# Attention in front of a mixture of experts: the next iteration's first scores and biases move ahead of the scaling and transposes of the second group

## What is computed

```python
# attention: batch 4, 8 heads, 576 tokens, head size 64; a window of 128 keys
scores = scale * np.matmul(q, k.transpose(0, 1, 3, 2))
bias = slopes[:, None, None] * (-np.abs(rel).astype(np.float32))[None, :, :]
mask = (rel >= 0) & (rel < window)
scores = np.where(mask, scores + bias[None], -1000000000.0)
attn = np.exp(scores - np.max(scores, axis=-1, keepdims=True))
attn = attn / (np.sum(attn, axis=-1, keepdims=True) + 1e-09)
x = np.matmul(attn, v)                      # then (2304, 512)
# mixture of experts: 8 experts, 512 -> 1024 -> 512, all of them for every token
P = np.exp(x @ w_gate - max); 8 rounds of row and column normalisation of P
for e in range(E):
    out += P[:, e:e + 1] * (np.maximum(x @ w1[e], 0.0) @ w2[e])
# feed-forward 512 -> 2048 -> 512 with a leaky relu
return np.maximum(0.01 * h, h) @ w_out      # h = out @ w_in
```

## Time and profile before

| | |
|---|---|
| median of 3 runs | 2029.84 us (2029.77 to 2029.85) |
| the profiled execution | 2029.62 us |
| its span, first to last instruction | 2027.8 us |
| mean granted clock of PE | 1.00 of full speed |
| busy: PE, DVE, ACT, POOL | 2013.9, 1196.0, 625.4, 1170.2 us |
| the chain that ended last: PE, DVE, ACT | 92%, 4%, 3% of the span |

### The profile page before, as it was taken

The page is one execution under the profiler, slowest core; times in us unless marked ns, Lnnn a source line. Parts: engine busy times, 40 slices in busy tenths (PEclk is TensorE's granted clock), DMA queues, the critical chain, the costliest instruction groups (busy, mean ns, idle before and its releaser), DMA issues.

```text
span 2027.8 us, 36541 instructions
## 1 busy us (share of the span) xinstructions
PE 2013.9 (99%) x12584; PEld 1791.1 (88%) x12584; DVE 1196.0 (59%) x2764; ACT 625.4 (31%) x1678; POOL 1170.2 (58%) x1453
## 2 busy tenths in 40 slices
PE   8999999999999999999999999999999999999999
PEld 6679889999998999989899999999999989998998
DVE  7877866555555455566555555555555577667666
ACT  7872232222222222232222222222222243334332
POOL 4425555555565665576555566655555576667551
PEclk9999999999999999999999999999999999999999
DMA  5311111111111111114211111111111115111211
GB/s 175 119 64 43 42 46 49 44 50 41 41 42 51 42 49 44 42 41 117 72 42 52 41 42 41 41 52 41 52 42 41 41 46 128 57 52 56 75 42 47
DMA packets 79891, 113.81 MB, mean 56 GB/s; under 512 B 44352, under 2 KB 53056, under 8 KB 79808
## 3 DMA queue, kind: packets, MB, share of 16 engines
q1 hardware_dynamic: 79808, 112.76, 17.7%
HBM read 103.30 MB, written 9.44 MB: 56 GB/s over the span
## 4 chain that ended last, share of the span: by engine, by line
PE 92%; DVE 4%; ACT 3%; issue 1%; POOL 0%; ACTq 0%; POOLq 0%; DVEq 0%
PE bank L1405 16%; PE bank L1406 16%; PE bank L1407 16%; PE bank L1324 14%; PE bank L1321 14%; PE bank L1323 14%; ACT sc L609 3%; DVE sc L847 1%; DVE sc L832 1%; ACT pt_sb L623 1%; DVE acc L931 0%; DVE row_sum L951 0%; DVE einv L843 0%; DVE esum_eps L841 0%; DVE lt_in L865 0%
## 5 line engine op out<-in xcount | busy, mean ns | idle before, releaser
L942 DVE SCALAR_TENSOR_TENSOR acc<-bank,gate,acc 128x512 f32<-128x512 f32 x495 | 371.6, 751 | 569.2 <-PE bank L1407 569.2
L1324 PE MATMUL bank<-x_hi,up_lo 128*128 128x256 f32 (+1 forms) x2240 | 663.0, 296 | 0.0
L1323 PE MATMUL bank<-x_lo,up_hi 128*128 128x256 f32 (+1 forms) x2240 | 662.4, 296 | 0.0
L1321 PE MATMUL bank<-x_hi,up_hi 128*128 128x256 f32 (+1 forms) x2240 | 661.0, 295 | 0.5 <-DVE hs_lo L1071 0.2
L1406 PE MATMUL bank<-down_lo,hs_hi 128*128 128x512 f32 x1440 | 568.0, 394 | 0.0
L1405 PE MATMUL bank<-down_hi,hs_hi 128*128 128x512 f32 x1440 | 567.5, 394 | 0.4 <-DVE hs_lo L1077 0.4
L1407 PE MATMUL bank<-down_hi,hs_lo 128*128 128x512 f32 x1440 | 560.2, 389 | 0.0
L1321 PEld LDWEIGHTS bank<-x_hi,up_hi 128*128 128x128 f32 x2240 | 423.9, 189 | 30.8 <-DVE bank L1055 1.6
L1323 PEld LDWEIGHTS bank<-x_lo,up_hi 128*128 128x128 f32 x2240 | 423.9, 189 | 24.6
L1324 PEld LDWEIGHTS bank<-x_hi,up_lo 128*128 128x128 f32 x2240 | 423.8, 189 | 0.0
L436 POOL TENSOR_TENSOR up_lo<-stage_up,up_hi 128x256 fp32r<-128x256 f32 x546 | 385.6, 743 | 6.3
(11 more groups left out here) (130 smaller groups left out, 1764.2 us busy)
## 6 DMA issues: line engine op xcount, KB each, us to landing
stage_up<-w_up SPq DMA_DIRECT2D x80, 512.0 KB, 3.5
stage_down<-w_down SPq DMA_DIRECT2D x80, 512.0 KB, 3.5
qk<-qk SPq DMA_DIRECT2D x15, 576.0 KB, 3.7
v_nat<-v SPq DMA_DIRECT2D x16, 320.0 KB, 2.9
x_mem<-x_turned SPq DMA_DIRECT2D x72, 64.0 KB, 2.2
xr<-x_mem SPq DMA_DIRECT2D x16, 256.0 KB, 4.7
result<-acc SPq DMA_DIRECT2D x16, 256.0 KB, 2.7
xr<-x_mem SPq DMA_DIRECT2D x4, 128.0 KB, 4.3
```

Of the source, the lines that this page charges most:

```text
L942: last = d.scalar_tensor_tensor(out=to, in0=y[:, :], scalar=share(g, tile, e), in1=to, op0=ALU.mult, op1=ALU.add)
L1321: m.matmul(to[:, 0:n], up_hi[s][:, w], x_hi[u][:, x], start=first and c == 0, stop=False, skip_group_check=True)
L1323: m.matmul(to[:, 0:n], up_hi[s][:, w], x_lo[u][:, x], start=False, stop=False, skip_group_check=True)
L1324: last = m.matmul(to[:, 0:n], up_lo[s][:, w], x_hi[u][:, x], start=False, stop=c == 1, skip_group_check=True)
```

## The change

Three things change, in the attention iterations alone.

- On PE, S0(i+1) moves from behind T0(i) to directly behind S2(i), ahead of V1(i-1) and T0(i). In iteration 0 twelve keep-busy steps become eight.
- On DVE, B0(i+1) moves from behind N1(i) (and behind the copy of the half logits and, in the last iteration, `sums`) to directly behind B2(i), ahead of N1(i).
- On POOL, `at(i, 0)` waits for N0(i-1) where it waited for N1(i-1). The waits of the groups 1 and 2 stay.

No instruction is added or removed apart from the four keep-busy steps, and ACT's and SP's lists stay as they are. Counts on the semaphores stay the same, since the order among the S, among the B and among the N is kept.

```diff
@@ POOL, at(i, group) @@
-                pool.wait_ge(normed, GROUPS * i + group - 1)
+                pool.wait_ge(normed, GROUPS * i + (-2, 0, 1)[group])
@@ DVE, step @@
                 bias_scores(i, 2, s, pair)
+                if not last:
+                    bias_scores(i + 1, 0, 1 - s, after)
                 normalise(i, 1, s)
                 if half is not None:
                     copy_lt_in(s, half)
                 if last:
                     sums(0, 2)
-                if not last:
-                    bias_scores(i + 1, 0, 1 - s, after)
                 normalise(i, 2, s)
                 if not last:
                     bias_scores(i + 1, 1, 1 - s, after)
@@ PE, step @@
                 scores(i, 2, s)
                 if first:
-                    keep_busy(12)
+                    keep_busy(8)
+                if not last:
+                    scores(i + 1, 0, 1 - s)
                 if not first:
                     values(i - 1, 1, 1 - s)
                 pe.wait_ge(normed, GROUPS * i + 1)
                 transpose_p(0, s)
-                if not last:
-                    scores(i + 1, 0, 1 - s)
                 if not first:
                     values(i - 1, 2, 1 - s)
```

## The result

The changed kernel takes 2038.65 us (median of 6 runs, 2036.78 to 2040.93) against 2029.80 us before: 8.85 us or 0.44% slower, ratio 1.0044 with a 95% interval of 1.0032 to 1.0057. The forecast was 2036.9, in a range of 2032.0 to 2041.6. The profiled execution took 2038.64 us with a span of 2036.9, 9.1 more than before.

A forecast was written before the change was run, and what follows sets the result against it. Attention was taken as bound by a ring of waits E0, C1, E1, N1, B0, replaced by one through B0 of 7.70 us. 107.8 + 1.7 logits + 4.1 POOL, with edges, gave +7.1 us: 2036.9, range 2032.0 to 2041.6.

The forecast's parts named there:

- a second ring that B0 joins: Attention: B1, N0, B2, B0, N1, T1, S1 across DVE and PE; 7.70 us a turn, 6.59 without B0.
- fourteen turns of the ring: Attention, S1 of iteration 1 to S1 of iteration 15: 14 x 7.70 = 107.8 us, against 106.6 before.
- logits ahead of S0: PE: logits queued before S0 make it late by some 0.5 us in iterations 6, 10, 14, 0.1 twice after: +1.7 us.
- POOL at N1: DVE: running POOL instructions hold back N1's L841 through the shared port; sum 3.7 to 4.6 us, taken as 4.1.
- the clock: PE idle before T1 might drop the clock to 1.2 GHz: +5 us per such turn, 2050 with two or three; chance 0.05.
- start, end: Attention's edges: S0 and B0 ahead of iteration 0's N1 cost +0.7 us; N1's shorter ACT wait in iteration 15 gives -0.6.
- rival 1: Attention: the port shared by POOL and DVE costs nothing; +3.0 us, 2032.9; chance 0.18.
- its two cases: Iterations 11 to 13: POOL's third instruction and L841 come due within 0.02 us of each other; 0.3 to 0.6 us each.
- A sign: DVE in attention: no idle ahead of N1, but some 0.9 us ahead of B1, released by PE.
- S0's place, the logits copy, E1 and ACT's slack: Attention: S0 has 0.6 us slack, the copy lies beside T1 and S1, E1 and ACT are in time; no cost.
- Rival 2: Attention: the gain comes through, ACT's 6.85 us a turn decides; -10.6 us at most, 2024.5 at half; chance 0.07.

The follow-up runs named there:

- the runs without POOL's hold: Changed kernel with POOL's groups of index 0 waiting for N2, not N0, of the previous iteration: 2033.28 us; the same plus matmuls filling PE's hole ahead of T1: 2034.76 us.
- the experiment on the kernel before: Kernel before with only POOL's wait changed, groups of index 0 let go behind N0 of the previous iteration: 2036.20 us, 6.6 slower, ratio 1.0033.
- the lightly filled kernel: Changed kernel with unread matmuls ahead of T1: seven steps in iteration 0, three in iterations without logits beside them, none in the others: 2036.86 us.
- PE's part alone: Kernel before with only S0 moved behind S2 and eight keep-busy steps, DVE's and POOL's lists as before: 2029.54 us, ratio 1.0000.
- the kernel with S1 early: Changed kernel with the next iteration's S1 ahead of T1 on PE and the half logits copy ahead of N1 on DVE: 2022.64 us, ratio to before 0.9965.
- the late POOL groups: Changed kernel with POOL's groups of index 0 waiting for N2 of the previous iteration instead of N0: 2033.28 us, ratio to before 1.0020.
- DVE's part alone: Kernel before with only B0 moved ahead of N1 on DVE, S0 still behind V1 and T0 on PE: 2079.81 us, ratio 1.0239.
- the three filled kernels: Changed kernel with unread matmuls ahead of T1: seven then four steps, 2037.70 us; fewer steps, 2036.86; seven then four plus POOL's index 0 groups behind N2, 2034.76.
- four more ahead of the hole: Changed kernel with twelve keep-busy steps, as before the change, instead of eight: 2040.81 us, 2.2 slower than the changed kernel.

## Why the prediction was right, point by point

The measured time lies in the range, and the mechanism, a second ring that B0 joins, is shown. The terms, for the fourteen turns between S1 of iteration 1 and S1 of iteration 15 and for what lies outside them, in us:

| term | forecast | profiled execution |
|---|---|---|
| fourteen turns of the ring | 107.8 | 107.9 |
| logits ahead of S0 | 1.7 | 0.75 |
| POOL at N1 | 4.1 | 4.1 |
| the clock | 0 | most of 2.5 left over |
| the fourteen turns | 113.6 | 115.2 |
| start, end | +0.7, -0.6 | +1.06, -0.68 |

- **The ring.** Seven terms from rows of before gave 7.70 us; the rows of after give 7.72, the runs without POOL's hold 7.71. By itself it costs 1.4 us over before, not the +3.0 of rival 1, which counts the logits too. One reading of before was off: five of the fourteen turns hold the logits copy, not six; the sixth lies behind them. The sum uses the measured 106.6 and is not touched.
- **The logits ahead of S0.** They were put at 1.7 us and cost 0.75: S0 is late by half of what was expected in iterations 6, 10 and 14, and not at all in 7 and 11.
- **POOL.** Expected 4.1 us; the steps from N1 to T1 hold 4.1 more than plain ones. It was put down from one held L841; the experiment on the kernel before shows the same wait alone at 6.6 us. In single iterations the guess was looser: iteration 2 came out at 0.2 and not 0.4, 10 and 14 at 0.3 and not 0.1; iteration 11, at 0.76 of L841, is the upper of its two cases.
- **The start.** Expected +0.7 at S1 of iteration 1; it starts at 14.67 and not 13.61, +1.06. B0 began at 10.84 instead of 10.6, and N1's L841 was held to 0.25 by POOL's first piece, which the sum had given 0.
- **The end.** N1 of iteration 15 waits 0.53 us for ACT instead of 1.12, and the last turn is 7.20 instead of 7.88: 0.7 given back, 0.6 expected.
- **The clock** is the term that the sum lacked. It stood as a rival with 0.05 and was said to be unlikely since every stretch of before is at 1.00. The rival's condition, holes of 1.1 to 1.8 us ahead of T1, came about, and behind two holes, one of them longer still, it fell. Its price was too high: about 2 us in sum (span 2036.9 against 2034.9 in the lightly filled kernel, 1.5 to 1.8 by the medians) and not 5 a turn, as a slow stretch lasts some 3 us and part of its slower matmuls lies in PE's own holes.
- **Luck.** The forecast's 2036.9 and the lightly filled kernel's 2036.86 look like a perfect sum with the clock alone missing. They are not: the logits were 1.0 us too high, and the start and POOL (4.3 to 4.5 in that kernel) too low by about as much together. With the logits right and no clock term the forecast would have been about 2036, further from the 2038.65 measured.
- **A sign.** DVE idles 1.42 us ahead of B1 in a plain turn, not the 0.9 named: N2 takes 0.70 us, and the 1.00 in the forecast had its wait in it. It changes no sum, as N2 lies beside T1 and S1.
- **S0's place, the logits copy, E1 and ACT's slack** were costed at nothing. PE's part alone (+0.0) shows it for S0; that DVE waits for ACT once only shows it for E1.
- **Rival 2, the gain.** It did not come, and the reason given (DVE's order is fixed) was true but not the whole of it: its order need not change. PE's S1 behind T1 closes the ring, and taking it out (the run also moved the copy of the half logits) gives the gain. The bound of 7.61 - 6.85 per turn was fair, the kernel with S1 early gets to 7.12.

## What to carry to other kernels

Filling an idle hole with work taken from the critical ring helps only if that work does not join the next ring: before moving it, add up every closed path through the new order, across engines, with start-to-start times from the trace, and compare the longest with the period of now. Here the second ring was 6.59 us without the moved step and 7.70 with it, against 7.48; moving the step that tied PE to the end of the ring, and the copy, turned 8.8 us lost into 6.9 gained. A total that fits doesn't show that its terms do: compare the start-to-start steps one by one, in every turn, before a difference between runs is given a name. When helper work on POOL is let go by a semaphore, place it beside VectorE operations that it does not exclude, and check after each change of order that it still falls there.

## What the runs showed of the hardware

- Exclusion between POOL and a small VectorE operation has no proportion to the latter's size: a 128x4 TENSOR_SCALAR took 1.02 us instead of 0.17 because a POOL cast had begun 0.03 us before it. Bias operations of 128x256 are at 0.41 or 0.42 us in every run of this case, beside POOL or not.
- Holes of 1.74 and 2.05 us on PE were followed by stretches of some 3 us at half clock, one of 1.75 us was not, and which executions had them varied: with the late POOL groups six of ten stood at 1.000. The kernel with S1 early has a hole of 1.72 us and no fall. In DVE's part alone a hole of 2.25 us stands in a long stretch at full clock:

```profile
26.09 1.09 PE L1248 MATMUL bank<-ident,sc 128*128 128x128 f32 x8 [2.25 <-DVE sc L847]
```

```profile
19.00:35.00 16.00, 11.25 (x152) 7.77 (x148) 12.03 (x68) 12.45 (x43) 4.02 (x5) 1.00 0.34 108
```

  So the length of the hole does not decide alone; what does stays open. Where all holes inside attention were at most 1.4 us, no profiled execution fell. A handful of matmuls that nothing reads, put in the hole itself, left all twenty executions of the three filled kernels at 1.00; four more ahead of the hole did not help.
- The clock can multiply a loss of waiting: DVE's part alone has two turns of 9.19 us, both at full clock, and mostly 10 to 14 us as run, with the clock at 0.61 to 0.92 in stretches of 20 us.
